# Low halves of rows before the weight maxima, and GpSimd's maximum between two groups of scatters

## The reference

```python
out = np.einsum('hk,bskhg->bshg', w, x_unf)          # convolution
logits = x @ w_gate
expert_idx = np.argmax(logits, axis=1)
gate_w = probs[np.arange(N), expert_idx]
for e in range(E):
    h = np.maximum(xe @ w1[e], 0.0)
    out[mask] = gate_w[mask, None] * (h @ w2[e])
# the second layer is the same, with a further factor
# 1 / (1 + exp(-(x @ w_output_gate))) of the chosen expert
```

## Time and profile before

| what | us |
|---|---|
| median of 3 runs | 1354.1 |
| lowest and highest | 1354.05, 1354.81 |
| the profiled execution | 1355.4 |
| its span, first to last instruction | 1353.8 |
| PE busy in it | 1214.6 |
| DVE busy in it | 869.7 |
| POOL busy in it | 451.5 |

### The profile page before, as it was taken

The page is one execution under the profiler, slowest core; times in us unless marked ns, Lnnn a source line. Parts: engine busy times, 40 slices in busy tenths (PEclk is TensorE's granted clock), DMA queues, the critical chain, the costliest instruction groups (busy, mean ns, idle before and its releaser), DMA issues.

```text
span 1353.8 us, 38270 instructions
## 1 busy us (share of the span) xinstructions
PE 1214.6 (90%) x13162; PEld 1092.6 (81%) x13162; DVE 869.7 (64%) x2322; ACT 638.7 (47%) x1126; POOL 451.5 (33%) x480
## 2 busy tenths in 40 slices
PE   3777683099999999999999999999999999999998
PEld 2666673088888888889999998888899999899997
DVE  3798887348999999997777777633433334333333
ACT  2676674135555555654444544433333333333342
POOL 1187777503333443332222222422222222222222
PEclk9666665599999999999999999999999999999999
DMA  8388856646876677553522246356442244262220
GB/s 231 90 261 272 254 191 193 212 99 160 228 191 159 160 195 206 140 150 84 130 50 55 54 102 147 74 148 166 109 110 61 56 103 106 57 164 59 55 52 17
DMA packets 237528, 181.20 MB, mean 134 GB/s; under 512 B 183263, under 2 KB 215675, under 8 KB 233890
## 3 DMA queue, kind: packets, MB, share of 16 engines
q1 hardware_dynamic: 209760, 114.76, 34.5%
q0 software_dynamic: 26096, 64.50, 15.6%
q10 hardware_dynamic: 1618, 1.26, 0.3%
HBM read 79.36 MB, written 70.80 MB: 111 GB/s over the span
## 4 chain that ended last, share of the span: by engine, by line
PE 56%; DVE 20%; issue 9%; DMA 7%; SPq 5%; ACT 2%; POOL 1%; DVEq 1%; ACTq 0%; POOLq 0%
PE bank L791 55%; DMA stage<-in_moe_w 5%; DVE hl L1214 2%; DVE wam L1090 2%; DVE split L1105 2%; DVE am L1021 1%; PE bank L796 1%; DVE xsl L1025 1%; DVE split L1108 1%; ACT rowt L642 1%; DMA wslot<-image 1%; POOL rows L531 1%; DVE rowab L1030 1%; DVE rowt L1030 1%; SPq L395 1%
## 5 line engine op out<-in xcount | busy, mean ns | idle before, releaser
L791 PE MATMUL bank<-xT,wslot 128*128 128x256 f16 (+1 forms) x5040 | 596.1, 273 | 40.3 <-DMA xT<-rows 33.7
L1214 DVE SCALAR_TENSOR_TENSOR hl<-bank,hh 128x512 f16<-128x512 f32 x504 | 347.6, 690 | 364.5 <-ACT hh L732 359.1
L791 PE MATMUL bank<-wslot,hh 128*128 128x192 f16 x4032 | 541.3, 246 | 0.0
L732 ACT ACTIVATE hh<-bank 128x512 f16<-128x512 f32 x504 | 300.6, 596 | 497.9 <-PE bank L791 488.9
L791 PEld LDWEIGHTS bank<-xT,wslot 128*128 128x128 f16 (+1 forms) x5040 | 420.3, 97 | 112.1 <-DMA xT<-rows 33.8
L791 PE MATMUL bank<-wslot,hl 128*128 128x192 f16 x2016 | 496.4, 246 | 0.0
L791 PEld LDWEIGHTS bank<-wslot,hh 128*128 128x128 f16 x4032 | 361.5, 98 | 28.4 <-issue 19.8
L611 POOL DMA_INDIRECT out_tokens<-y,idxt x126 | 122.8, 974 | 370.5 <-ACT y L744 323.6
L552 POOL DMA_INDIRECT rows<-rowt,idxp x126 | 133.2, 1057 | 338.7 <-PE bank L791 210.5
L791 PEld LDWEIGHTS bank<-wslot,hl 128*128 128x128 f16 x2016 | 197.4, 98 | 0.0
L642 ACT ACTIVATE rT<-bank 128x672 f16<-128x672 f16 (+1 forms) x127 | 97.9, 773 | 69.6 <-PE bank L796 69.5
(11 more groups left out here) (145 smaller groups left out, 873.7 us busy)
## 6 DMA issues: line engine op xcount, KB each, us to landing
wslot<-image SPq DMA_DIRECT2D x20, 1024.0 KB, 5.6
wslot<-image SPq DMA_DIRECT2D x20, 768.0 KB, 4.7
image<-split POOLq DMA_DIRECT2D x18, 512.0 KB, 4.8
image<-split SPq DMA_DIRECT2D x8, 1024.0 KB, 4.4
image<-split POOLq DMA_DIRECT2D x9, 768.0 KB
xw<-in_x SPq DMA_DIRECT2D x4, 1536.0 KB, 11.5
stage<-in_moe_w SPq DMA_DIRECT2D x8, 768.0 KB, 10.2
image<-split SPq DMA_DIRECT2D x8, 768.0 KB, 6.2
```

The costliest lines, as they stand in the source:

```text
L732: nc.scalar.activation(hh[:, c, :], bank[c][:, :], ACT.Relu).then_inc(hh_out, 1)
L791: return nc.tensor.matmul(o, a, b_, start=start, stop=stop, skip_group_check=True)
L1214: V.scalar_tensor_tensor(hl[:, c, :], bank[c][:, :], 0.0, hh[:, c, :], ALU.max, ALU.subtract).then_inc(hl_out, 1)
```

## The change

Two places change. In VectorE's step the first maximum of the weights (`weights_max(..., 0)`) moves from ahead of the low halves of the rows to behind them, so that both maxima stand together. In GpSimd's step the scatters are issued in two groups of eight, with `weight_maxima` between them, where all sixteen stood ahead of it. No instruction is added or taken out.

```diff
             def step(n, b, q):
                 if late(n, 1):
-                    scatter_step(n - 1)
+                    scatter_step(n - 1, 0)
                 weight_maxima(n, q)
+                if late(n, 1):
+                    scatter_step(n - 1, 1)
...
-            def scatter_step(n):
-                pool.wait_ge(index_ready, n + 1)
-                pool.sem_inc(pool_turn, 1)
-                for w in range(G):
+            def scatter_step(n, half):
+                if half == 0:
+                    pool.wait_ge(index_ready, n + 1)
+                    pool.sem_inc(pool_turn, 1)
+                for w in range(half * G // 2, (half + 1) * G // 2):
...
             steps(pool, step)
-            scatter_step(STEPS - 1)
+            for half in range(2):
+                scatter_step(STEPS - 1, half)
...
-                weights_max(q, stage_loaded[q], (b + 1) * 64, 0)
                 dve.wait_ge(hi_ready, n + 1)
                 row32 = rowa[n % SLOTS][0:WIN, :, :]
                 V.tensor_copy(row32[:, :, MI:MI + 1], ids[0:WIN, :].unsqueeze(2))
                 low_rows(xs[0:WIN, :, :], row32.bitcast(f16)).then_inc(lo_ready, 1)
+                weights_max(q, stage_loaded[q], (b + 1) * 64, 0)
                 weights_max(q, None, None, 1)
```

## The result

The changed kernel takes **1336.4 us** (median of 4 runs, 1336.13 to 1337.59), the kernel before 1354.45 us on the same chip (4 runs, 1354.05 to 1355.08). The ratio is 0.9868, with a 95% interval of 0.9851 to 0.9885: 1.3% faster, some 18 us. The forecast was 1343.0 us, with a range of 1338.5 to 1348.

The account below looks back on a forecast made before the run. Once the `stage` waits go, GpSimd's scatter pace was taken to bound the start of the expert phase: 12.1 us of index waits less 1.0 of gaps gives 11.1, so 1354.1 - 11.1 = 1343.0 us, range 1338.5 to 1348.

Parts of the forecast that it names:

- The wait for `stage` and the step: VectorE's convolution steps: waits for `stage` fall from 16.4 to under 4 us, steps from 26.0 to 23.3 to 24.0.
- Denser DMA traffic: Rival, chance 0.04: denser traffic delays the `stage` load and the kernel gets slower, 1360 us if the load takes 19 us.
- VectorE's side: VectorE's index path to the last scatters: last index 15 to 19 us earlier; as a rival bounding the kernel, chance 0.15.
- GpSimd's idle time: GpSimd's scatters: 12.1 us of index waits go, 1.0 us of gaps stays, so the last scatter is issued 11.1 us earlier.
- The reduction in the middle: GpSimd's reduction between two groups of eight scatters waits for nothing, and VectorE's 1.3 us wait for the maxima goes.
- The holds: GpSimd's scatters held beside VectorE's two-tile instructions: 3.3 us a step, unchanged, give or take 4 us in all.
- The rival of shrinking holds: With one more reduction between low halves, fewer scatters are caught: end 15 us earlier, 1338 to 1340 us; chance 0.13.
- the row load moves with the scatters: Start of the expert phase: first row load keeps following the last scatter by 5 us, the rest behind it unchanged.
- a sign of being wrong: Listed sign that the prediction fails: the first row load doesn't follow the last scatter by 5 us.
- VectorE isn't blocked: Beside GpSimd's scatters VectorE isn't slowed: low halves of rows last 1.22 us with GpSimd idle and with scatters running.
- the rival: Nothing gained, chance 0.06: scatters block VectorE's four two-tile instructions, 3.8 us a step, step 27 us, 1352 to 1356 us.
- The margins: Index against GpSimd: the index a step before the last is 9.9 to 13.3 us earlier, GpSimd 9 to 10.

Follow-up runs that it names:

- the repeats: The changed kernel run again unchanged, twice, in other runs: 1337.8 us (ratio 0.9871) and 1337.6 us (ratio 0.9867).
- VectorE's part alone: Changed kernel with all sixteen scatters again ahead of GpSimd's reduction, only VectorE's new order kept: 1342.7 us, ratio 0.9908.

## Why the prediction was right and wrong

- **The wait for `stage` and the step.** Right. Under 4 us were expected and 0.9 came; the step's own work was worked out as 23.3 us and is 23.1 to 23.4. Denser DMA traffic didn't delay the load, and the last index comes 21.3 us earlier (236.5 to 215.2), a little beyond the 15 to 19 us that VectorE's side was said to allow.
- **GpSimd's idle time.** Right to the tenth in this profile: 12.1 - 1.0 = 11.1 us forecast, 49.0 - 38.0 = 11.1 measured, 10.6 and 11.2 in the repeats. The step on which the forecast rests held.
- **The reduction in the middle.** Right. It never waits, and `wmx` is ready early; without the split 9.7 us of waits return and 5 us of the gain go, part of them at the landing.
- **The holds.** Here the prediction failed: a term of its sum was mis-sized. It was put at 3.3 us a step, unchanged, with 4 us either way; it fell from 28.0 to 23.6 us, by 4.4 (2.9 in the two repeats). For the low halves of the weights this could be worked out from rows of before: a scatter stands 0.72 us into L1105, scatters come every 1.25 us, and the edit moves L1105 by the 2.2 us of one reduction against them, which puts one at 0.72 - 2.2 + 2.5 = 1.02 us; 1.01 was measured. The rival of shrinking holds named the sign and gave it 0.13, as if it excluded the likeliest case; the two add up.
- **The end.** The second step that failed is "the row load moves with the scatters", 5 us behind the last one: it comes 3.6 us behind, 1.5 less, in the repeats too. The prediction had named this as a sign of being wrong. The last scatter now lands in 1.8 us of waiting instead of 3.3. In the thirteen profiles this wait goes with how long before the last scatter SyncE issued the first expert weights (L404): 4.7 us at 1.7 us before; 3.3 and 3.6 at 3.2 and 3.3; 2.8 and 2.6 at 5.0 and 5.1; 1.8 each time at 6.5 or more. The two are seen together; nothing was run that moves that load alone. The prediction read that the load would move by 15 us or more (it went 21.2 us earlier, to 234.65) and drew no gain from it.
- **The start.** 1.9 us are chance, in this profile and in no repeat by as much (0.0 and 0.8). By terms that repeat the gain is 15 to 17 us, by the ratios 17.5 to 18.0. Whether the ratios hold some of this chance too, or a difference in the expert phase, is not settled; it is a rest of 1 to 3 us.
- **VectorE isn't blocked.** Right for the two-tile instructions, on which the rival rested: L1033 lasts 1.21 and L1034 2.28 us beside scatters in the changed kernel as well, and none in any trace is longer by more than 0.08 us. Too strong as a general statement: VectorE's nine scalings of rows (L1136) take 2.15 us with GpSimd idle and 2.3 beside scatters in the kernel before, and 3.13 beside the memset on GpSimd. By the Trainium skill (SBUF - State Buffer, "Who interferes with whom") whichever engine issues first blocks the other. The traces agree with the order: a scatter begun 0.10 us behind L1109 (217.99 against 217.89) goes free, and L1109 then lasts 2.42 instead of 2.34 us; one begun 0.12 us behind the same instruction in the kernel with VectorE's part alone is held for 2.1 us. What they don't show beside a scatter is VectorE blocked for the scatter's length. The Trainium skill's statement (same section) that a reduction doesn't contend agrees: no scatter of the changed kernel is held by L1094 or L1096.
- **The margins.** The prediction called the one of steps 1 to 6 thin, and then let GpSimd's pace alone count. That was right for its sum and too simple for what comes next: 0.73 us a step more on VectorE cost 4.6 us, and 7 us less of holds, paid for with 0.46 us a step on VectorE, brought nothing.

## What to carry to other kernels

When two engines fill a step between them, work out both loops, and then each term of the time from the last common point to the end: start, idle time, stalls inside instructions, landing. An edit that shifts two engines' instructions against each other moves their mutual stalls as well, so a stall that recurs in each period is to be worked out again from the new phase and not carried over. After a gain like this, lengthen each engine by a little in turn; where both cost their full price, shortening one alone can bring little. And when stalls in one kind of instruction fall, look whether another kind has taken them over.

## What the runs showed of the hardware

- A scatter's issue can be held through three instructions of VectorE in a row, 4.95 us, and comes free beside a reduction; cut into pieces of 0.6 to 1.4 us the same work holds 16.4 us instead of 23.6 to 25.1, and takes VectorE 0.46 us a step more.
- A reduction over the partitions on GpSimd is held like a scatter: 1.12 to 2.14 us instead of 0.32 beside VectorE's low halves of the weights.
- Where a scatter stands when VectorE's instruction begins decides its hold: begun 0.23 us ahead or 0.10 us behind it goes free, begun 0.12 us behind it is held 2.1 us, begun 0.72 and 1.01 us behind it 1.5 and 1.2 us.
- A tensor_scalar of VectorE with one input tile, at 1.1 us for 2048 columns, holds a scatter too (0.69 and 0.38 us).
- A `memset` of 1.02 us on GpSimd cost 1.5 to 1.7 us a step, since the next scatter then came 0.81 instead of 0.16 us behind; where it fell beside nine tensor_scalars of VectorE, these took 3.13 us instead of 2.15 (seen once).
- The last scatter lands after 1.8 us of waiting when the weight load was issued 6.5 us or more before it, and after 3.3 to 4.7 when 1.7 to 3.3 us before (seen together, not intervened on).
- One and the same round of float32 matmuls took 4.4 to 5.5 us from execution to execution, at a granted clock of 0.64 to 0.50 of full speed, and the first scatter came up to 3 us later with it.
